# Expert weights stored in four 5 KB runs per partition, one store on another queue, two units loaded and squared earlier

## The chip, the cores and the metric

The kernel runs on one NeuronCore of a Trainium2 chip as one program. Its time is the device time in microseconds; of the kernel before there are three runs, median 822.89 us (820.84 to 823.64).
## The reference

Three stages follow each other. A gated linear recurrence over 4 x 8 heads of 768 steps gives 3072 rows of 320 numbers. Each row goes through one of eight experts (two products with a relu between them, 320 to 1024 to 320), the one with the largest logit, and is scaled by its gate. Then a dense layer follows (320 to 2048 to 320).

```python
for t in range(S):                      # recurrence, for every batch and head
    m_new = np.maximum(f_gate[:, :, t] + m, i_gate[:, :, t])
    f_stab = np.exp(f_gate[:, :, t] + m - m_new)
    i_stab = np.exp(i_gate[:, :, t] - m_new)
    C = f_stab * C + i_stab * outer(v_t, k_t);  n = f_stab * n + i_stab * k_t
    y[:, :, t] = sigmoid(o_gate_t) * (C @ q_t) / max(abs(n . q_t), 1)
# experts
expert_idx = np.argmax(x @ w_gate, axis=1); gate_w = softmax(x @ w_gate)[expert_idx]
for e in range(8):
    out[mask] = gate_w[mask, None] * (np.maximum(x[mask] @ w1[e], 0) @ w2[e])
# dense layer
h = x @ w_in; g = np.maximum(0.01 * h, h); return g @ w_out
```

## The kernel before

Everything is in single precision at the borders; weights and activations of the experts and of the dense layer are split in two halves of 16 bits each (a high and a low part), and each product is made of three 16-bit products.

**The weights.** There are ten weight units: 0 to 7 are the experts in the order in which they will be used, 8 and 9 the two halves of the dense layer. A unit goes through four steps, always in five parts (three of its first matrix, two of its second): it is *loaded* as f32 into one half of `stage` (even units into half 0, odd ones into half 1); ACT *squares* each part and keeps the row sums (`square`); TensorE adds the sums over partitions (`sums`), and DVE makes the unit's scale from them (`scale`); ACT writes the *high* parts and DVE the *low* parts into one of four 16-bit buffers `slot0` to `slot3`. Units 0 and 1 stay in slots 0 and 1. Units 2 to 7 are built in other slots and *stored* to `d_w` in DRAM, 20 KB in each of 128 partitions: unit 2 and 3 in two pieces of 10 KB (`store_A`, `store_B` on the sync queue, during the recurrence), 4 to 7 in one piece (`store_unit` on ACT's queue). The sync engine fetches them back into slots 0 and 1 in two pieces of 10 KB per partition when the expert two before them is done (the last loop of the sync block).

**The pairs.** The expert stage walks 31 pairs (tile of 128 rows, expert), in the order of the experts. In step p TensorE makes the first product of pair p (`h_product`, 64 matmuls), the second of pair p - 1 (`y_product`, 24 matmuls), and turns the rows of pair p + 2 (`x_turn`, 3 matmuls). Both products stand twice in the code, for slot 0 and slot 1, behind a branch on the parity of the expert. ACT copies out the high parts (`h_high`, `x_high`), scales the next rows (`x_cast`); DVE makes the low parts (`h_low`, `x_low`), the scale of the rows (`x_scale`) and adds the result (`y_add`). GpSimd gathers the rows of later pairs.

**What sets the order.** The steps of the weight units are spread over the pairs by tables at the end of the file. `PAIR_SQ` names the squares that ACT does in `jobs(p)`, `PAIR_HI` the high parts there, `PAIR_LO` the low parts that DVE does in its `jobs(p)`, `PAIR_SCALE` the pair before which TensorE adds the sums (and DVE makes the scale), `PAIR_STORE` and `PAIR_LOAD` the pairs at whose end ACT issues a store or a load (`keep(p)`). On ACT a step p is `h_high(p)`, `jobs(p)`, `x_cast(p + 3)`, `x_high(p + 2)`, `keep(p)`; on DVE `h_low(p)`, `x_scale(p + 3)`, `jobs(p)`, `y_gate` and `y_add` of p - 1, `x_low(p + 2)`. A load of unit x waits until the low parts of unit x - 2 are made, since they read the same half of `stage`. TensorE's pairs are loops of two pairs each, cut at the keys of `PAIR_SCALE` (3 to 9, 9 to 13, 13 to 23, 23 to 29). After the pairs comes the dense layer, six groups of four tiles, in which nothing of this is left but the two units in slots 2 and 3.

Of the kernel before, what the change touches and what calls it, by code (L numbers as in the profile page):

```python
# [24 lines left out]
F16 = mybir.dt.float16  # L25
# [8 lines left out]
P = 128  # L34
# [14 lines left out]
NF = FE // P  # L49
# [15 lines left out]
def build(nc, qkT, k_in, v_in, o_in, ig, fg, wg_in, wA, wB, out):  # L65
    ctx = ExitStack()
    with ctx:
# [3 lines left out]
        def dram(name, shape, dt):  # L71
            return nc.dram_tensor(name, shape, dt, kind="Internal").ap()
# [4 lines left out]

        d_parts = dram("d_parts", (6, BH, S), BF16)
        d_wl = dram("d_wl", (BH, NC), F32)
        d_w = dram("d_w", (NE, P, 5 * FE + NF * 2 * DM), F16)  # L80
        d_x = dram("d_x", (NTOK, DM), F32)

        slot = [sb(f"slot{i}", [P, 5 * FE + NF * 2 * DM], F16) for i in range(4)]
        slotA = [t[:, 0:5 * FE] for t in slot]
        slotB = [t[:, 5 * FE:] for t in slot]
# [100 lines left out]
        hi_done, lo_done = sem("hi_done"), sem("lo_done")  # L187
        stored = [sem(f"stored{k}") if k >= 2 else None for k in range(NE)]
# [9 lines left out]
        wA_landed = [sem(f"wA_landed{i}") for i in range(2)]  # L198
        wB_landed = [sem(f"wB_landed{i}") for i in range(2)]
# [120 lines left out]
        def _(sp):  # L320
# [13 lines left out]
            def load_B(x):  # L334

                h = x % 2
                r = row_of(sp, x)
                sp.dma_start(stB[h].rearrange("p (m e) -> p m e", m=NF // 2),
                             wB[ds(r, 1)].rearrange("a (m p r) d -> p (a m) (r d)", m=NF // 2, p=P)).then_inc(stgB_landed[h], 16)

            def store_A(x):

                sp.wait_ge(lo_done, lows_until(x, 3))
                sp.dma_start(d_w[x - 2, :, 0:5 * FE], slotA[SLOT[x]][:, :]).then_inc(stored[x], 16)

            def store_B(x):

                sp.wait_ge(lo_done, lows_until(x))
                sp.dma_start(d_w[x - 2, :, 5 * FE:], slotB[SLOT[x]][:, :]).then_inc(stored[x], 16)

            def load_k(c, b):
                i = buf(c, b)
# [37 lines left out]
            for g in range(NG):  # L390
                r = heads(g) * D
# [80 lines left out]
            sp.wait_ge(lo_done, lows_until(1))  # L472
            load_A(5)
            load_B(5)
            sp.wait_ge(rt_tab, 1)
            for e in range(2, NE):
                last = sp.value_load(tab_last[0:1, e - 2:e - 1], min_val=0, max_val=NPAIR)
                sp.wait_ge(stored[e], stores(e))
                sp.wait_ge(m_h, 2 * (last + 1))
                sp.dma_start(slotA[e % 2][:, :], d_w[e - 2, :, 0:5 * FE]).then_inc(wA_landed[e % 2], 16)  # L480
                sp.wait_ge(m_o, last + 1)
                sp.dma_start(slotB[e % 2][:, :], d_w[e - 2, :, 5 * FE:]).then_inc(wB_landed[e % 2], 16)

        @block.gpsimd
# [215 lines left out]
        def _(act):  # L701
# [188 lines left out]
            def store_unit(x):  # L890

                act.wait_ge(lo_done, lows_until(x))
                act.dma_start(d_w[x - 2], slot[SLOT[x]][:, :]).then_inc(stored[x], 16)

            def x_high(p, i):
                act.wait_ge(mtr, p + 1)
# [603 lines left out]
        def _(pe):  # L1500
# [373 lines left out]
SLOT = (0, 1, 0, 1, 2, 3, 2, 3, 2, 3)  # L1874
# [28 lines left out]
PAIR_LO = {0: ((4, 0), (4, 1)), 1: ((4, 2), (4, 3)), 2: ((4, 4), (5, 0)), 3: ((5, 1), (5, 2)), 4: ((5, 3), (5, 4)),  # L1903
# [90 lines left out]
```

## Time and profile before

| | |
|---|---|
| median of 3 runs | 822.89 us |
| the profiled execution | 821.72 us |
| its span | 820.0 us |
| TensorE busy | 748.0 us, 91% |
| VectorE (DVE) busy | 518.3 us, 63% |
| ScalarE (ACT) busy | 415.9 us, 51% |
| GpSimd (POOL) busy | 192.4 us, 23% |
| DMA | 95.77 MB in 35879 packets |

The profiled execution took 1.17 us less than the median. The recurrence lies at about 12 to 190 us of the span, the choice of experts at 190 to 217, the pairs at 217 to 465, and the dense layer from there to the end. In the page a group of rows names line, engine, operation, what is written and read, and how often; "issue" is time in which an engine waited for nothing that the profile shows; ACTq and SPq are the sequencers of ACT and SP, on which DMAs are issued.

### The profile page before, as it was taken

To read this page: it belongs to the slowest core of one execution; us is meant where nothing else is said; L and a number is where in the kernel's file an instruction comes from. 1 tells how busy PE (TensorE), PEld (TensorE's weight loads), DVE (VectorE), ACT (ScalarE), POOL (GpSimd) and SP (SyncE) were. 2 spreads that over 40 slices of the span, in tenths; PEclk is the share of its full clock that TensorE was granted. 3 is DMA by queue.
4 is the path that set the end of the run, shared out by engine and by line. 5 is a ranking of instruction groups with operands and counts; after the bars stand their busy time and mean duration, and the time that the engine had idled before them with its cause. 6 is when DMAs were issued, how large, how long until landed. Compare 5 with 4: busy or idle time off the path is not lost.

```text
span 820.0 us, 17971 instructions
## 1 busy us (share of the span) xinstructions
PE 748.0 (91%) x6435; PEld 554.9 (68%) x6436; DVE 518.3 (63%) x1346; ACT 415.9 (51%) x811; POOL 192.4 (23%) x286
## 2 busy tenths in 40 slices
PE   4899999993697989799999899999999999999994
PEld 3688889882486878687888756556565555565552
DVE  7868898997876545565567665555465455554441
ACT  4578777778652266554656223343443433434332
POOL 4468787782311001010100000020010100100101
PEclk9999999997798989999999999999999999999997
DMA  6889979732415974478330000000000000000000
GB/s 198 225 233 298 335 239 318 226 128 80 127 59 215 354 253 147 162 282 338 109 139 0 2 1 1 1 33 1 1 33 1 33 0 0 32 0 0 33 2 32
DMA packets 35879, 95.77 MB, mean 117 GB/s; under 512 B 7102, under 2 KB 19582, under 8 KB 33246
## 3 DMA queue, kind: packets, MB, share of 16 engines
q1 hardware_dynamic: 28434, 63.71, 24.6%
q10 hardware_dynamic: 4732, 22.10, 7.5%
q0 software_dynamic: 2640, 9.01, 3.3%
q8 instruction: 43, 0.70, 0.4%
q14 instruction: 30, 0.25, 0.1%
HBM read 70.92 MB, written 23.89 MB: 116 GB/s over the span
## 4 chain that ended last, share of the span: by engine, by line
PE 79%; DVE 5%; ACT 5%; DMA 4%; issue 4%; SPq 1%; POOL 1%; ACTq 0%; DVEq 0%; POOLq 0%
PE bank L1669 33%; PE bank L1806 19%; PE bank L1703 10%; PE bank L1532 4%; PE bank L1556 4%; DMA stage<-wA 2%; ACT xw L777 1%; PE bank L1578 1%; PE bank L1542 1%; PE bank L1548 1%; PE bank L1659 1%; DMA slot<-qkT 1%; DMA d_x<-og 1%; PE bank L1522 1%; PE bank L1524 1%
## 5 line engine op out<-in xcount | busy, mean ns | idle before, releaser
L1669 PE MATMUL bank<-stage,slot 128*128 128x512 f16 x768 | 181.1, 379 | 0.0
L1806 PE MATMUL bank<-slot,dec 128*128 128x320 f16 x768 | 159.1, 299 | 0.0
L1669 PE MATMUL bank<-qbd,slot 128*128 128x128 f16 x1984 | 122.5, 225 | 13.7 <-issue 9.3
L1669 PEld LDWEIGHTS bank<-qbd,slot 128*128 128x128 f16 x1984 | 118.4, 101 | 17.2 <-issue 16.8
L1669 PEld LDWEIGHTS bank<-stage,slot 128*128 128x128 f16 x768 | 75.1, 98 | 74.3 <-DVE stage L1464 0.3
L1468 DVE TENSOR_TENSOR qk<-stage,dec 128x512 f16<-128x512 f32 x96 | 66.4, 692 | 85.1 <-ACT dec L964 85.1
L1806 PE MATMUL bank<-slot,qk 128*128 128x320 f16 x384 | 114.8, 299 | 0.0
L964 ACT CAST dec<-stage 128x512 f16<-128x512 f32 x96 | 59.4, 619 | 101.1 <-PE bank L1806 74.5
L693 POOL DMA_INDIRECT out<-stage,tok_i x24 | 23.6, 983 | 369.5 <-ACT stage L975 365.6
L1464 DVE TENSOR_TENSOR stage<-bank,stage 128x512 f32<-128x512 f32 x96 | 66.2, 690 | 67.0 <-ACT stage L958 66.0
L958 ACT ACTIVATE stage<-bank 128x512 f32<-128x512 f32 x96 | 57.3, 597 | 97.2 <-PE bank L1669 96.2
L1703 PE MATMUL bank<-slot,emov 128*128 128x320 f16 x496 | 102.0, 299 | 4.3 <-DVE esta L1364 2.4
L1806 PEld LDWEIGHTS bank<-slot,dec 128*128 128x128 f16 x768 | 75.1, 98 | 44.3 <-DVE qk L1468 0.2
L905 ACT ACTIVATE emov<-bank 128x512 f16<-128x512 f32 x62 | 36.8, 597 | 92.0 <-PE bank L1669 88.5
L1703 PE MATMUL bank<-slot,esta 128*128 128x320 f16 x248 | 74.2, 299 | 0.0
L1364 DVE SCALAR_TENSOR_TENSOR esta<-bank,emov 128x512 f16<-128x512 f32 x62 | 42.1, 689 | 47.2 <-ACT emov L905 46.8
L1125 DVE SCALAR_TENSOR_TENSOR slot<-stage,wsc,slot 128x1024 f16<-128x1024 f32 (+2 forms) x50 | 71.0, 1430 | 0.4
L793 ACT ACTIVATE slot<-stage,wsc 128x1024 f16<-128x1024 f32 (+1 forms) x50 | 62.2, 1276 | 0.7 <-DVE winvp L1105 0.7
L1703 PEld LDWEIGHTS bank<-slot,emov 128*128 128x128 f16 x496 | 46.9, 98 | 22.1 <-issue 5.6
L1806 PEld LDWEIGHTS bank<-slot,qk 128*128 128x128 f16 x384 | 37.6, 98 | 14.6
L1132 DVE TENSOR_TENSOR dec<-bank,dec 128x384 f32<-128x384 f32 (+1 forms) x72 | 36.4, 506 | 14.4 <-ACT dec L835 13.5
L607 POOL TENSOR_TENSOR own<-state,bdm 120x123 f32<-120x123 f32 x60 | 41.6, 705 | 5.7 <-PE bank L1548 4.7
(268 smaller groups left out, 1187.6 us busy)
## 6 DMA issues: line engine op xcount, KB each, us to landing
slot<-d_w SPq DMA_DIRECT2D x12, 1280.0 KB, 6.5
d_w<-slot ACTq DMA_DIRECT2D x4, 2560.0 KB, 11.2
stage<-wB SPq DMA_DIRECT2D x6, 1280.0 KB, 9.0
stage<-wA SPq DMA_DIRECT2D x6, 1024.0 KB
d_w<-slot SPq DMA_DIRECT2D x4, 1280.0 KB, 8.3
stage<-wB ACTq DMA_DIRECT2D x4, 1280.0 KB, 13.2
qk<-qkT SPq DMA_DIRECT2D x12, 360.0 KB, 5.9
slot<-qkT SPq DMA_DIRECT2D x12, 360.0 KB, 7.8
```

The costliest lines, as they stand in the source:

```text
L607: nc.gpsimd.tensor_tensor(own[u % 3][0:GH * D, :], state[0:GH * D, b, g, :], bdm[0:GH * D, :], ALU.mult).then_inc(st_own, 1)
L793: a.activation(o_, t, ACT.Copy, scale=sc).then_inc(hi_done, 1)
L905: a.activation(hh[i][:, q * 512:(q + 1) * 512], bank[2 * i + q][:, :], ACT.Relu).then_inc(m_hh, 1)
L958: a.activation(ft[f % 2], bank[f % 2][:, :], ACT.Copy, scale=0.01).then_inc(f_t, 1)
L964: a.copy(fhi[f % 2], fgl[f % 2]).then_inc(f_hi, 1)
L1125: v.scalar_tensor_tensor(o_, x, sc, h_, ALU.mult, ALU.subtract).then_inc(lo_done, 1)
L1364: v.scalar_tensor_tensor(hl[i][:, q * 512:(q + 1) * 512], bank[2 * i + q][:, :], 0.0, hh[i][:, q * 512:(q + 1) * 512], ALU.max, ALU.subtra ...
L1464: v.tensor_tensor(fgl[f % 2], bank[f % 2][:, :], ft[f % 2], ALU.max).then_inc(f_g, 1)
L1468: v.tensor_tensor(flo[f % 2], fgl[f % 2], fhi[f % 2], ALU.subtract).then_inc(f_lo, 1)
L1669: ins = t_.matmul(pf, a[:, col:col + P], x(k), start=(q == 0), stop=(q == len(ops) - 1))
L1703: ins = t_.matmul(bank[4 + i][:, 0:DM], x[i][:, f * P:(f + 1) * P], slotB[s][:, c0:c0 + DM], start=(f == 0 and q == 0), stop=(f == NF - 1 ...
L1806: ins = t_.matmul(bank[4 + q][:, 0:DM], x[f % 2][:, q * P:(q + 1) * P], slotB[2 + f // NF][:, c0:c0 + DM], start=(f == 0 and z == 0), stop ...
```

## The change

Three things change. `d_w` is laid out as four runs of 2560 numbers (5 KB) per partition, all partitions of a run together, and each store and each fetch back moves rows of 5 KB (`WRUN`, `in_runs`, `kept`). The store of unit 4 goes from ACT's `keep(2)` to the sync engine, ahead of its fetches. The tables move the steps of units 4 to 8.

```diff
-        d_w = dram("d_w", (NE, P, 5 * FE + NF * 2 * DM), F16)
+        d_w = dram("d_w", (NE, 4, P, WRUN), F16)
...
+        def in_runs(t):
+            return t.rearrange("p (r w) -> p r w", w=WRUN)
+        def kept(e, lo, hi):
+            return d_w[e - 2, lo:hi].rearrange("r p w -> p r w")
...
                 sp.wait_ge(lo_done, lows_until(x, 3))
-                sp.dma_start(d_w[x - 2, :, 0:5 * FE], slotA[SLOT[x]][:, :]).then_inc(stored[x], 16)
+                sp.dma_start(kept(x, 0, 2), in_runs(slotA[SLOT[x]])).then_inc(stored[x], 16)
...
                 sp.wait_ge(lo_done, lows_until(x))
-                sp.dma_start(d_w[x - 2, :, 5 * FE:], slotB[SLOT[x]][:, :]).then_inc(stored[x], 16)
+                sp.dma_start(kept(x, 2, 4), in_runs(slotB[SLOT[x]])).then_inc(stored[x], 16)
...
             load_A(5)
             load_B(5)
+            sp.wait_ge(lo_done, lows_until(4))
+            sp.dma_start(kept(4, 0, 4), in_runs(slot[SLOT[4]])).then_inc(stored[4], 16)
             sp.wait_ge(rt_tab, 1)
             for e in range(2, NE):
                 last = sp.value_load(tab_last[0:1, e - 2:e - 1], min_val=0, max_val=NPAIR)
                 sp.wait_ge(stored[e], stores(e))
                 sp.wait_ge(m_h, 2 * (last + 1))
-                sp.dma_start(slotA[e % 2][:, :], d_w[e - 2, :, 0:5 * FE]).then_inc(wA_landed[e % 2], 16)
+                sp.dma_start(in_runs(slotA[e % 2]), kept(e, 0, 2)).then_inc(wA_landed[e % 2], 16)
                 sp.wait_ge(m_o, last + 1)
-                sp.dma_start(slotB[e % 2][:, :], d_w[e - 2, :, 5 * FE:]).then_inc(wB_landed[e % 2], 16)
+                sp.dma_start(in_runs(slotB[e % 2]), kept(e, 2, 4)).then_inc(wB_landed[e % 2], 16)
...
             def store_unit(x):
                 act.wait_ge(lo_done, lows_until(x))
-                act.dma_start(d_w[x - 2], slot[SLOT[x]][:, :]).then_inc(stored[x], 16)
+                act.dma_start(kept(x, 0, 4), in_runs(slot[SLOT[x]])).then_inc(stored[x], 16)
...
-PAIR_SCALE = {9: 6, 13: 7, 23: 8}
+PAIR_SCALE = {9: 6, 15: 7, 23: 8}
...
-PAIR_STORE = {2: 4, 4: 5, 13: 6, 17: 7}
-PAIR_LOAD = {5: 6, 8: 7, 14: 8, 18: 9}
+PAIR_STORE = {4: 5, 13: 6, 18: 7}
+PAIR_LOAD = {3: 6, 6: 7, 14: 8, 18: 9}
```

`PAIR_SQ`, `PAIR_HI` and `PAIR_LO` change with them. The squares of unit 6 go from pairs 7 (three) and 8 (two) to pairs 5, 6 (two each) and 7 (one); those of unit 7 from pairs 11 (two) and 12 (three) to one in each of the pairs 9 to 13; those of unit 8 from pairs 16 and 17 to 17, 18 and 19. The high parts of unit 7 go from pairs 13 to 15 to 15 to 17, its low parts from 14 to 17 to 15 to 18. Of unit 4's low parts four now lie in pair 0 (before: two) and the fifth in pair 1 (before: pair 2).

What stands on ACT before, from the load of unit 6 at the end of pair 5 (rows `DMA stage<-wA`) to the squares of that unit (`xw,sq<-stage`) in pairs 7 and 8. Each pair begins with `emov<-bank 128x512` (`h_high`) and has `qk<-` (`x_cast`) and `qbd<-bank` (`x_high`).

```order
L883 DMA stage<-wA 128x2x1024
L886 ISA
L886 DMA stage<-wA 64x1024 x2
L887 DMA stage<-wB 128x4x640
L905 ACTIVATE emov<-bank 128x512 [waits m_h] x2
L920 ACTIVATE qk<-num,sxs 128x320 [waits mtr,xs_scale]
L921 ACTIVATE qk<-num,sxs 128x64
L899 CAST qbd<-bank 128x384 [waits m_h,mtr]
L905 ACTIVATE emov<-bank 128x512 [waits m_h] x2
L777 ACTIVATE xw,sq<-stage 128x1024 [waits sq_done,stgA_landed0]
L777 ACTIVATE xw,sq<-stage 128x1024 [waits sq_done] x2
```

The same stretch of ACT in the changed kernel: the load of unit 6 at the end of pair 3, the store of unit 5 at the end of pair 4, and the first squares in pair 5.

```order
L893 DMA stage<-wA 128x2x1024
L896 ISA
L896 DMA stage<-wA 64x1024 x2
L897 DMA stage<-wB 128x4x640
L915 ACTIVATE emov<-bank 128x512 [waits m_h] x2
L930 ACTIVATE qk<-og,sxs 128x320 [waits mtr,xs_scale]
L931 ACTIVATE qk<-og,sxs 128x64
L909 CAST qbd<-bank 128x384 [waits m_h,mtr]
L903 DMA d_w<-slot 128x4x2560 [waits lo_done]
L915 ACTIVATE emov<-bank 128x512 [waits m_h] x2
L787 ACTIVATE xw,sq<-stage 128x1024 [waits sq_done,stgA_landed0]
L787 ACTIVATE xw,sq<-stage 128x1024 [waits sq_done]
```

One whole pair lies between the load and the first square in both; the store of unit 5, which stood before the load, now stands behind it in ACT's queue.

On ACT before pair 13, before: the squares of unit 7 in pairs 11 and 12, ahead of the high parts of the same unit (`slot<-stage`, waiting for its scale, `sc_chain`) in pair 13.

```order
L777 ACTIVATE xw,sq<-stage 128x1024 [waits sq_done,stgA_landed1]
L777 ACTIVATE xw,sq<-stage 128x1024 [waits sq_done]
L920 ACTIVATE qk<-og,sxs 128x320 [waits mtr,xs_scale]
L921 ACTIVATE qk<-og,sxs 128x64
L899 CAST qbd<-bank 128x384 [waits m_h,mtr]
L905 ACTIVATE emov<-bank 128x512 [waits m_h] x2
L777 ACTIVATE xw,sq<-stage 128x1024 [waits sq_done]
L777 ACTIVATE xw,sq<-stage 128x1280 [waits sq_done,stgB_landed1]
L777 ACTIVATE xw,sq<-stage 128x1280 [waits sq_done]
```

In the changed kernel, from the last square of unit 7 in pair 13 to its first high part in pair 15:

```order
L787 ACTIVATE xw,sq<-stage 128x1280 [waits sq_done]
L930 ACTIVATE qk<-num,sxs 128x320 [waits mtr,xs_scale]
L931 ACTIVATE qk<-num,sxs 128x64
L909 CAST qbd<-bank 128x384 [waits m_h,mtr]
L903 DMA d_w<-slot 128x4x2560 [waits lo_done]
L915 ACTIVATE emov<-bank 128x512 [waits m_h] x2
L930 ACTIVATE qk<-num,sxs 128x320 [waits mtr,xs_scale]
L931 ACTIVATE qk<-num,sxs 128x64
L909 CAST qbd<-bank 128x384 [waits m_h,mtr]
```

A pair now lies between the last square and the sum that TensorE makes of them, where before the sum stood right behind it.

On DVE in pairs 0 and 1, before: the low parts of units 4 and 5 (`slot<-stage,wsc,slot`), the gates of the pairs (`gmt<-bank`), and `x_low` of pair 2 (`qbd<-bank,qbd`), for which TensorE's pair 2 waits.

```order
L1354 RECIPROCAL sxs<-sxi 128x1 [waits xs_chain]
L1125 SCALAR_TENSOR_TENSOR slot<-stage,wsc,slot 128x1024 [waits hi_done] x2
L1320 TENSOR_REDUCE gmt<-bank 128x31 [waits rt_gate]
L1359 TENSOR_TENSOR qbd<-bank,qbd 128x384 [waits m_xh,rt]
L1364 SCALAR_TENSOR_TENSOR esta<-bank,emov 128x512 [waits m_hh] x2
```

And in the changed kernel:

```order
L1135 SCALAR_TENSOR_TENSOR slot<-stage,wsc,slot 128x1024 [waits hi_done] x2
L1135 SCALAR_TENSOR_TENSOR slot<-stage,wsc,slot 64x1024 [waits hi_done]
L1135 SCALAR_TENSOR_TENSOR slot<-stage,wsc,slot 128x4x320 [waits hi_done]
L1330 TENSOR_REDUCE gmt<-bank 128x31 [waits rt_gate]
L1369 TENSOR_TENSOR qbd<-bank,qbd 128x384 [waits m_xh,rt]
L1374 SCALAR_TENSOR_TENSOR esta<-bank,emov 128x512 [waits m_hh] x2
```

Two more low parts stand ahead of the gates and of `x_low`.

## Rows read from the trace of the kernel before

**Rows 1.** The page: busy times and the granted clock in 40 slices.
```profile
PE 748.0 (91%) x6435; PEld 554.9 (68%) x6436; DVE 518.3 (63%) x1346; ACT 415.9 (51%) x811; POOL 192.4 (23%) x286
PEclk9999999997798989999999999999999999999997
```
**Rows 2.** Timeline of PE, clean pairs: start, duration, operation, count, idle before.
```profile
352.08 3.74 PE L1669 MATMUL bank<-qbd,slot 128*128 128x128 f16 x64 [0.21 <-issue]
...
373.72 3.74 PE L1669 MATMUL bank<-qbd,slot 128*128 128x128 f16 x64
```
**Rows 3.** Timeline of PE, pairs 2 to 6 and 8 to 9.
```profile
234.72 0.49 PE L1659 MATMUL bank<-ident,qk 128*128 128x128 f32 x3
...
242.20 3.74 PE L1669 MATMUL bank<-qbd,slot 128*128 128x128 f16 x64
...
253.73 6.07 PE L1669 MATMUL bank<-qbd,slot 128*128 128x128 f16 x64 [4.20 <-issue]
...
271.78 3.75 PE L1669 MATMUL bank<-qbd,slot 128*128 128x128 f16 x64 [0.88 <-issue]
...
286.16 3.74 PE L1669 MATMUL bank<-qbd,slot 128*128 128x128 f16 x64
...
295.04 0.36 PE L1591 MATMUL bank<-sq,onesf 128*128 128x5 f32 x2 [1.55 <-ACT xw L777]
297.23 6.49 PE L1669 MATMUL bank<-qbd,slot 128*128 128x128 f16 x64 [1.83 <-DVE qbd L1359]
```
**Rows 4.** Timeline of PE, pairs 12 to 14 and 19.
```profile
323.21 3.74 PE L1669 MATMUL bank<-qbd,slot 128*128 128x128 f16 x64
...
334.06 5.20 PE L1669 MATMUL bank<-qbd,slot 128*128 128x128 f16 x64 [2.09 <-DVE qbd L1359]
...
348.11 0.44 PE L1703 MATMUL bank<-slot,emov 128*128 128x320 f16 x2 [1.69 <-DVE esta L1364]
...
382.74 3.75 PE L1669 MATMUL bank<-qbd,slot 128*128 128x128 f16 x64 [1.70 <-issue]
```
**Rows 5.** Timeline of ACT: first and last of four stores, load and square of unit 6.
```profile
243.57 0.36 ACTq L893 DMA_DIRECT2D d_w<-slot  x1
...
250.47 0.46 ACT L899 CAST qbd<-bank 128x384 f16<-128x384 f32 x1
...
272.47 0.45 ACTq L883 DMA_DIRECT2D stage<-wA  x1
...
286.71 1.06 ACT L777 ACTIVATE xw<-stage 128x1024 bf16<-128x1024 f32 x1 [3.33 <-DMA stage<-wA]
...
374.29 0.34 ACTq L893 DMA_DIRECT2D d_w<-slot  x1
```
**Rows 6.** DMA view: packets, and issues with sizes and time to landing.
```profile
DMA packets 35879, 95.77 MB, mean 117 GB/s; under 512 B 7102, under 2 KB 19582, under 8 KB 33246
...
q8 instruction: 43, 0.70, 0.4%
q14 instruction: 30, 0.25, 0.1%
...
slot<-d_w SPq DMA_DIRECT2D x12, 1280.0 KB, 6.5
d_w<-slot ACTq DMA_DIRECT2D x4, 2560.0 KB, 11.2
```
**Rows 7.** Windows: busy times, granted clock, DMA share, GB/s.
```profile
250.00:260.00 10.00, 6.27 (x67) 6.20 (x68) 4.13 (x6) 1.69 (x5) 0.94 (x1) 0.66 0.51 197
280.00:290.00 10.00, 10.00 (x143) 9.05 (x140) 3.90 (x11) 4.42 (x7) 0.10 (x1) 1.00 1.01 358
```
**Rows 8.** Timeline of DVE, pairs 0 and 1: low parts, `x_low` of pair 2.
```profile
227.39 2.46 DVE L1125 SCALAR_TENSOR_TENSOR slot<-stage,wsc,slot 128x1024 f16<-128x1024 f32 x2
...
231.91 0.56 DVE L1359 TENSOR_TENSOR qbd<-bank,qbd 128x384 f16<-128x384 f32 x1 [0.70 <-ACT qbd L899]
...
234.84 2.87 DVE L1125 SCALAR_TENSOR_TENSOR slot<-stage,wsc,slot 64x1024 f16<-64x1024 f32 x2
```

More of the change, by code:

```diff
@@ L1857 @@
 NBUF = 4
+WRUN = 2560
 EARLY = 4
@@ L1894 @@
 STABLE = {(1, 0): (1, 2), (1, 1): (2, 3), (1, 2): (3, 4), (2, 0): (4, 5), (2, 1): (5, NC)}
-PAIR_SQ = {7: ((6, 0), (6, 1), (6, 2)), 8: ((6, 3), (6, 4)),
-           11: ((7, 0), (7, 1)), 12: ((7, 2), (7, 3), (7, 4)), 16: ((8, 0), (8, 1)), 17: ((8, 2), (8, 3), (8, 4)),
-           20: ((9, 0), (9, 1), (9, 2)), 21: ((9, 3), (9, 4))}
-PAIR_SCALE = {9: 6, 13: 7, 23: 8}
+PAIR_SQ = {5: ((6, 0), (6, 1)), 6: ((6, 2), (6, 3)), 7: ((6, 4),),
+           9: ((7, 0),), 10: ((7, 1),), 11: ((7, 2),), 12: ((7, 3),), 13: ((7, 4),), 17: ((8, 0),), 18: ((8, 1), (8, 2)),
+           19: ((8, 3), (8, 4)), 20: ((9, 0), (9, 1), (9, 2)), 21: ((9, 3), (9, 4))}
+PAIR_SCALE = {9: 6, 15: 7, 23: 8}
 PAIR_HI = {0: ((5, 0), (5, 1)), 1: ((5, 2), (5, 3)), 2: ((5, 4),),
[2 rows of a table removed]
[2 rows of a table added]
            23: ((8, 0), (8, 1)), 24: ((8, 2), (8, 3)), 25: ((8, 4), (9, 0)), 26: ((9, 1), (9, 2)), 27: ((9, 3), (9, 4))}
-PAIR_LO = {0: ((4, 0), (4, 1)), 1: ((4, 2), (4, 3)), 2: ((4, 4), (5, 0)), 3: ((5, 1), (5, 2)), 4: ((5, 3), (5, 4)),
+PAIR_LO = {0: ((4, 0), (4, 1), (4, 2), (4, 3)), 1: ((4, 4), (5, 0)), 2: ((5, 1), (5, 2)), 3: ((5, 3),), 4: ((5, 4),),
            9: ((6, 0),), 10: ((6, 1),), 11: ((6, 2),), 12: ((6, 3),), 13: ((6, 4),),
[1 row of a table removed]
[1 row of a table added]
            23: ((8, 0),), 24: ((8, 1), (8, 2)), 25: ((8, 3),), 26: ((8, 4), (9, 0)), 27: ((9, 1), (9, 2)),
            28: ((9, 3), (9, 4))}
-PAIR_STORE = {2: 4, 4: 5, 13: 6, 17: 7}
-PAIR_LOAD = {5: 6, 8: 7, 14: 8, 18: 9}
+PAIR_STORE = {4: 5, 13: 6, 18: 7}
+PAIR_LOAD = {3: 6, 6: 7, 14: 8, 18: 9}
 TOK_AT = 21
```

6 rows, old and new, of tables (PAIR_HI, PAIR_LO) are left out of this document.

## The prediction

> **What bounds the kernel now.** I read the page first, then the timeline of TensorE (PE) pair by pair, then the timelines of ACT and DVE where PE is late, and last the DMA view. PE is busy 91% of the span, and the row of granted clocks is full but for a dent between 180 and 330 us [rows 1]: what is lost lies in the expert stage, not in the dense layer. A clean pair, from the first product of pair 15 (352.08) to that of pair 18 (373.72), takes 21.64 / 3 = 7.21 us, in which the 64 matmuls of a first product take 3.74 [rows 2]. From pair 3 (242.20) to pair 18 there are 15 pairs; 131.52 - 15 x 7.21 = 23.4 us too many, and pair 19 waits 1.70 more: 25 us lost [rows 2 to 4]. They have two kinds of cause.
>
> **Two sums that wait for ACT.** Before pair 9 PE adds the squares of unit 6, and waits 1.55 us for them; the first product then starts another 1.83 us late, since PE came to its register work only behind that wait [rows 3]. Of ACT one sees why: the first square of unit 6 waited 3.33 us for a load that was issued at 272.47 and landed at 286.7, 14.2 us later [rows 5], with the DMA engines 101% busy from 280 to 290 [rows 7]. Pair 8 to 9 takes 297.23 - 286.16 = 11.07, 3.86 too many, and the product of pair 9 runs at the lower clock in part, 6.49 against 3.74, 2.75 more [rows 3]: 6.6 us. Before pair 13 the same with unit 7, whose squares stand in pair 12 itself: 334.06 - 323.21 = 10.85, 3.64 too many, and 5.20 against 3.74, 1.46 more [rows 4]: 5.1 us.
>
> **Four waits that no engine explains.** Pair 4 waits 4.20 us [rows 3], pair 6 0.88 [rows 3], the second product behind pair 14's first 1.69 and pair 19 1.70 [rows 4]; the releaser given for the third, a low part of pair 14, is none that `y_product(13)` waits for. Each begins 3 to 7 us after ACT issued one of its four stores (the first at 243.57, the last at 374.29 [rows 5], the others at 265.3 and 343.3): at 249.5, 270.9, 346.4 and 381.0. A store takes 11.2 us to land [rows 6], so all four lie inside one. Beside other traffic that keeps the DMA engines as busy, 280 to 290 at 1.01, PE is busy 10.00 of 10.00 [rows 7]. What the stores have that the rest lacks is rows of 20 KB: 35879 - 33246 = 2633 packets are of 8 KB or more, and 12 fetches, 4 stores of unit halves and 4 whole stores at 128 each make 2560 of them, the 43 + 30 instruction fetches the other 73 [rows 6]. An instruction fetch is 0.70 MB / 43 = 16 KB in one packet [rows 6]; both products stand behind a branch, so PE needs such fetches in every pair. I read the four waits as fetches, or register loads, held up behind 20 KB packets: 4.20 + 0.88 + 1.69 + 1.70 = 8.47 us. The longest cost the clock too: 0.66 of it granted from 250 to 260 [rows 7], partly at 1.2 GHz, and 64 matmuls in 6.07 instead of 3.74 [rows 3], 2.33 more. Together 10.8 us.
>
> On this the Trainium skill agrees in kind: "Runtime: NRT & Kernel Launch" (Instruction fetch mechanics) says that a taken branch out of the window stops the engine for a DMA fetch, and "DMA: Bandwidth & Descriptors" (Queues, rings and completion order) that a DMA engine changes queues only at packet boundaries. The second page's section "Issuing engines are not separate DMA queues" speaks against a part of this change: a store moved to another issuer runs on the same 16 engines and saves only issue time; by it the fifth unit's store on the sync queue is worth nothing for itself, and what it may bring is its earlier start. The sum below gives it nothing.
>
> **The change part by part.**
>
> *Squares of unit 6 two pairs sooner.* The load goes out at the end of pair 3, when `x_high(5)` is done, at 250.9 [rows 5]; its first square stands in pair 5. If pair 4 no longer waits (249.5), pair 5 starts at about 256.7, and ACT comes to the square behind its copy of the product, some 4.2 us later, at 260.9: 10 us after the issue. The load took 14.2 us where store 5's tail and two fetches ran beside it; now the fetch of unit 2 (issued about 246, 6.5 us to land) runs beside its start, and the store of unit 5, about 258, stands behind it in ACT's queue. I expect 9 to 12 us. ACT may wait 5 us more there without delaying PE: `x_high(7)` would be ready at about T5 + 8.1 and is needed at T5 + 14.3. So the point of no cost is a landing of 15 us. Sum 6 then needs nothing that isn't done 8 us earlier, and PE passes it as it passes other waits. Gain 6.6; from below, if the sum still waits, 0.
>
> *Squares of unit 7 spread over pairs 9 to 13, sum at pair 15.* The last lies one pair ahead of the sum. Each pair gets one square beside at most two high parts, on an ACT with room: what stood in a pair before (three squares) was more. Gain 5.1; nothing else in the pair is late behind it. The low parts end in pair 18 instead of 17, and store 7 and load 9 are issued one behind the other; unit 7 is fetched 5 pairs later and unit 9 squared 2 pairs later, so both have over 14 us.
>
> *Runs of 5 KB.* The number of bytes stays; 3584 packets are added (1536 for four whole stores, 512 for the halves, 1536 for the fetches). What a store of 5 KB rows costs PE is not in the trace. From above: the four waits stay, 0. From below: they go, with the clock, 10.8. The nearest row is the busy window with 10 KB rows and no wait [rows 7], nearer to the gain. I take a quarter of the waits as left, as the packet is a quarter as long: 3/4 x 8.47 + 2.33 = 8.7. A cost of more, smaller packets I put at 0: over half the packets are already under 2 KB [rows 6].
>
> *Unit 4's low parts and its store.* DVE makes four in pair 0, not two: one over 64 partitions and one of 1280 columns more, 2.87 us for the like pair [rows 8]. They end at 229.85 + 2.87 = 232.7; with the short sum of the gates behind them, `x_low(2)` starts at about 233.0 instead of 231.91 and ends at 233.6 [rows 8]. PE turns the next rows at 234.72 [rows 3]; 1.1 us are left. In pairs 1 and 2 DVE is as much behind and has as much left. Cost 0; without that cover 1 us a pair. The store starts at about 237.6 instead of 243.57 and has landed at 249 when pair 4 begins. The sync engine waits there for low parts; behind it stands only the fetch of unit 2, which must wait for pair 3 anyway (246).
>
> *What it adds.* Between 250 and 272 the load of unit 6, the store of unit 5 and the second fetch of unit 2 lie closer than before, with pairs 4 to 7 beside them. The 0.88 us of pair 6 is the nearest row for such a crowd [rows 3]; I add 1.0 us.
>
> **The sum**, from the profiled execution: 821.72 - 6.6 - 5.1 - 8.7 + 1.0 = 802.3 us. That execution lay 1.17 below the median of 822.89; against the median I predict 803.5 us.
>
> **Rivals.**
>
> 1. *The four waits stay.* They come from reading SBUF or from the branch, not from long rows. For it: pair 4 is the first that takes the other branch. Against it: pairs 11 and 18 switch too and don't wait. Only 6.6 + 5.1 go: 821.72 - 11.7 + 1.0 = 811.0, against the median 812.2.
> 2. *The load of unit 6 is late again, two pairs sooner.* The 3.33 us of ACT come back in pair 5 or 6, now beyond its 5 us of room, and a pair starts late with a slow product: 2 to 4 us and 2.8 us for the clock. 803.5 + 5 to 7 = 809 to 810.
> 3. *It gets slower.* One mechanism: rows of 5 KB slow load, store and fetch in the crowd of 250 to 272 so far that ACT stands in pair 5 at the first square. It costs nothing up to 15 us of landing and then its full excess, plus 2.8 us for the clock; it eats the 19.4 us of gain only from 15 + 16.6 = 32 us, over twice the 14.2 that the most crowded load took [rows 5]. Then 823 to 828.
> 4. *All four waits and the added crowd come to nothing:* 821.72 - 6.6 - 5.1 - 10.8 = 799.2, against the median 800.4.
>
> **How the numbers follow.** Forecast 0.58 (own range 800 to 807), rival 1 0.15, rival 2 0.12, rival 4 0.08, rival 3 0.04, and 0.03 that gains and new waits cancel to within 0.3% (2.5 us, about what a measurement of this kernel can tell). The range takes in rivals 1, 2 and 4: 798 to 813. Faster 0.93, same 0.03, slower 0.04.
>
> **What would show it.** Right: pair 9 and pair 15 (first product) start within 7.5 us of the one before, and no product of 64 matmuls from pair 4 to 18 takes over 4 us; the windows from 250 to 340 have a granted clock of 1.00; the four stores have no wait of PE over 1 us inside them; about 39460 packets, of which 73 of 8 KB or more. Wrong: a wait "issue" of several us near pair 4 with a store of 5 KB rows in flight (rival 1); an ACT square of unit 6 waiting for `stage<-wA` in pair 5 and a late pair 7 (rival 2); a load that needs over 20 us (rival 3). The recurrence and the dense layer should take as long as before; a gain there would be none of mine.

## The result: 0.7% faster, some 28% of the gain forecast

The changed kernel takes 818.18 us in the median of 9 runs (813.51 to 819.57), beside 823.64 for the kernel before on the same chip (820.84 to 827.13): a ratio of 0.9927, 95% interval 0.9906 to 0.9948. The forecast was 803.5 us, with a range of 798 to 813. Faster is right; it was to bring 19.4 us, and 5.5 came (823.64 less 818.18). The profiled execution has a span of 817.7 us. Lines of the changed kernel that stand behind the diff are 10 higher (`h_product` is L1679, `y_product` L1713).

From the page of the changed kernel, the rows that answer to [rows 1, 6]:

```profile
PE 747.7 (91%) x6435; PEld 552.2 (68%) x6436; DVE 518.1 (63%) x1346; ACT 415.4 (51%) x811; POOL 193.2 (24%) x286
...
PEclk9999999997799999989999999999999999999997
...
DMA packets 39463, 95.77 MB, mean 117 GB/s; under 512 B 7102, under 2 KB 19582, under 8 KB 39390
...
q8 instruction: 43, 0.70, 0.4%
q14 instruction: 30, 0.25, 0.1%
```

The packets are as forecast (39463, of them 73 of 8 KB or more). The dents of the clock in slices 13 and 15 (246 to 266 and 287 to 308 us) are gone, and a new one stands in slice 18, at 350 us. Where the time went is told best by the starts of the first products of the pairs, taken from the timeline of TensorE (PE), whose rows for the new trouble are these (start, duration, idle time before and its releaser):

```profile
246.73 3.75 PE L1679 MATMUL bank<-qbd,slot 128*128 128x128 f16 x64 [1.90 <-issue]
...
291.33 0.28 PE L1601 MATMUL bank<-sq,onesf 128*128 128x5 f32 x2
291.53 0.67 PE L1679 MATMUL bank<-qbd,slot 128*128 128x128 f16 x9
...
335.50 0.28 PE L1601 MATMUL bank<-sq,onesf 128*128 128x5 f32 x2
336.96 3.75 PE L1679 MATMUL bank<-qbd,slot 128*128 128x128 f16 x64 [1.18 <-issue]
...
345.80 3.75 PE L1679 MATMUL bank<-qbd,slot 128*128 128x128 f16 x64 [1.51 <-issue]
353.30 0.71 PE L1713 MATMUL bank<-slot,emov 128*128 128x320 f16 x2 [3.76 <-issue]
...
359.55 3.74 PE L1679 MATMUL bank<-qbd,slot 128*128 128x128 f16 x64
...
400.26 5.09 PE L1679 MATMUL bank<-qbd,slot 128*128 128x128 f16 x64 [1.40 <-DVE esta L1374]
```

Both sums are passed without a wait: unit 6 at 291.33 (1.55 and 1.83 us lost there before [rows 3]) and unit 7 at 335.50. But pairs 15 and 16 now wait three times, 1.18 + 1.51 + 3.76 = 6.45 us, and the longest wait costs the clock as well. Pair 3 waits 1.90 us where it waited for nothing before; this lies inside the 46.86 us of pairs 2 to 8 below. The windows of the changed kernel (busy times, granted clock, DMA share, GB/s):

```profile
345.00:350.00 5.00, 3.75 (x64) 3.58 (x64) 1.71 (x3) 1.02 (x2) 0.46 (x1) 1.00 0.99 307
350.00:355.00 5.00, 1.70 (x7) 1.02 (x8) 4.39 (x9) 3.21 (x5) 1.52 (x1) 0.69 0.07 21
355.00:360.00 5.00, 5.00 (x31) 3.25 (x29) 0.47 (x1) 0.25 (x1) 0.37 (x1) 0.62 0.11 33
```

PE was idle from 349.5 to 353.3 and then ran its second product with a granted clock of 0.62, 0.71 us for two matmuls where 0.43 is usual. The DMA engines were full until 350 (load of unit 8, issued 335.70) and all but empty after it.

A table from the starts of first products, in us; a clean pair is 7.21:

| from the start of pair to pair | before | after | forecast of the difference | difference |
|---|---|---|---|---|
| 2 to 8 | 51.12 | 46.86 | -5.1 (waits of pairs 4 and 6, clock, +1.0) | -4.26 |
| 8 to 11 | 29.88 | 22.45 | -6.6 (sum of unit 6) | -7.43 |
| 11 to 12 | 7.17 | 7.17 | 0 | 0 |
| 12 to 15 | 28.87 | 23.17 | -6.4 (sum of unit 7, wait in pair 14) | -5.70 |
| 15 to 18 | 21.64 | 29.75 | 0 | +8.11 |
| 18 to 23 | 38.06 | 42.23 | -1.3 (wait of pair 19) | +4.17 |
| 2 to 23 | 176.74 | 171.63 | -19.4 | -5.11 |

Up to pair 15 the change brought 17.4 us of 18.1. The miss lies behind it. (Pair 2 starts at 237.31, before at 235.04; over the traces of this study it lies between 235.0 and 239.6, and most of that arises ahead of the pairs, where traces of kernels with the same code differ by up to 4 us, so the rest of this text compares pairs 2 to 23, and medians. One part of it is the change's own: from the first product of pair 0 to that of pair 2 it is 14.47 us, before 14.03.)

### The profile page after: what moved, and what is told of

It reads as the page before. It is cut to its first block, busy times and chain, and to the rows that moved or that the text cites. A ratio compares the mean times of both kernels' runs of the same rounds, so it can differ in the third digit from the quotient of the medians.

```text
span 817.7 us, 17971 instructions
## 1 busy us (share of the span) xinstructions
PE 747.7 (91%) x6435; PEld 552.2 (68%) x6436; DVE 518.1 (63%) x1346; ACT 415.4 (51%) x811; POOL 193.2 (24%) x286
## 2 busy tenths in 40 slices
DMA packets 39463, 95.77 MB, mean 117 GB/s; under 512 B 7102, under 2 KB 19582, under 8 KB 39390
## 4 chain that ended last, share of the span: by engine, by line
PE 80%; DVE 7%; DMA 5%; issue 4%; ACT 2%; SPq 1%; POOL 1%; ACTq 0%; DVEq 0%; POOLq 0%
PE bank L1679 33%; PE bank L1816 19%; PE bank L1713 11%; PE bank L1542 4%; PE bank L1566 4%; DMA stage<-wA 2%; PE bank L1588 1%; PE bank L1552 1%; PE bank L1558 1%; PE bank L1669 1%; DMA slot<-qkT 1%; DMA d_x<-og 1%; PE bank L1532 1%; PE bank L1534 1%; PE bank L1793 1%
## 5 line engine op out<-in xcount | busy, mean ns | idle before, releaser
L1679 PE MATMUL bank<-stage,slot 128*128 128x512 f16 x768 | 181.1, 379 | 0.0
L1679 PE MATMUL bank<-qbd,slot 128*128 128x128 f16 x1984 | 117.5, 220 | 10.0 <-issue 8.3
L1679 PEld LDWEIGHTS bank<-stage,slot 128*128 128x128 f16 x768 | 75.1, 98 | 74.3 <-DVE stage L1474 0.2
L1679 PEld LDWEIGHTS bank<-qbd,slot 128*128 128x128 f16 x1984 | 113.2, 98 | 13.9 <-issue 13.5
L1713 PE MATMUL bank<-slot,emov 128*128 128x320 f16 x496 | 104.3, 304 | 7.0 <-issue 6.3
L1713 PE MATMUL bank<-slot,esta 128*128 128x320 f16 x248 | 75.3, 304 | 0.0
L1713 PEld LDWEIGHTS bank<-slot,emov 128*128 128x128 f16 x496 | 47.6, 99 | 26.2 <-issue 8.7
```

Source lines behind the costliest of these rows:

```text
L1679: ins = t_.matmul(pf, a[:, col:col + P], x(k), start=(q == 0), stop=(q == len(ops) - 1))
L1713: ins = t_.matmul(bank[4 + i][:, 0:DM], x[i][:, f * P:(f + 1) * P], slotB[s][:, c0:c0 + DM], start=(f == 0 and q == 0), stop=(f == NF - 1 ...
```

## The theory: new code under full DMA engines

PE's program holds four copies of the pair loop, since each sum of squares ends one loop and starts the next: pairs 3 to 8, 9 up to the sum of unit 7, on to 22, and 23 on. Theory N: PE fetches its code only where it has not run yet, so in the first pass (two pairs) of each copy; if the DMA engines are full then, that fetch is late, whatever the row length. Moving the sum of unit 7 from pair 13 to 15 moved the start of the third copy onto the load of unit 8, issued at 335.70. The DMA view, cut to windows, shows the code packets of PE's queue (q8). From 332 to 356 us of the changed kernel:

```profile
q8 instruction: 3, 0.05, 0.9%
```

and none from 356 to 400, while the five pairs 17 to 21 run, in which only the second instruction queue, q14 [rows 6], has a packet:

```profile
q14 instruction: 1, 0.01, 0.0%
```

The view puts a packet where it starts. In narrow windows the three start at 342.3, 350.2 and 353.4. The first two belong to waits of PE, the one that ends at 345.80 and the one that ends at 353.30; the third starts when PE is already running again. Each wait goes on for some 2 us behind its packet (of about 1 us), the longest with the DMA engines all but empty (share 0.07 from 350): the full engines can have made that packet late, but not the time behind it.

The rivals were the prediction's term C (the rows decide), and R: a full DMA system stops PE in any pass. No packet of q8 lies near the first wait (1.18 us, ahead of pair 15; none from 304.5 to 342): theory N doesn't explain it, and it comes back below.

## Experiments

Ratios are to the kernel before on the same chip, with 95% intervals. "Time 2 to 23" is from the first product of pair 2 to that of pair 23, in the profiled execution.

**1. The rows alone** (e1_runs_alone), on the kernel before: `d_w` in runs of 5 KB, with `kept` and `in_runs` for stores and fetches.

> The kernel before with the 5 KB rows and nothing else. Theory N (the waits are fetches of TensorE's own code, which happen only in the first two pairs of each of the four copies of the pair loop, and last long when the DMA engines are full, whatever the rows): the waits before h_product of pairs 4, 10, 13/14 stay in sum within 3 us of the 8.5 us of before, and the time is 0.998 to 1.004 of before. The prediction's term C (row length sets the waits): at least three of the four waits fall under 1 us, and the time is 0.987 to 0.993 of before.

Measured: 821.68 us, 0.9974 (0.9953 to 0.9996). Ahead of pair 4, timeline of PE:

```profile
255.45 5.37 PE L1677 MATMUL bank<-qbd,slot 128*128 128x128 f16 x64 [3.87 <-issue]
```

3.87 us where it was 4.20 [rows 3]; pair 14 waits 1.09 (1.69 [rows 4]) and pair 19 1.69 (1.70). Pairs 2 to 8 take 50.18 us (51.12), all other stretches the same within 0.06. Rows of 5 KB are worth about 1 us in the trace and, by the interval of the ratio, 0.3 to 3.9 us in the time, not 8.7. The ratio lies between the two forecasts, 0.0006 outside theory N's and further from term C's; only one wait of four is under 1 us (pair 6, 0.58, before 0.88), where term C wanted three.

**2. The changed kernel with the old rows** (e2_long_rows):

```diff
-        d_w = dram("d_w", (NE, 4, P, WRUN), F16)
+        d_w = dram("d_w", (NE, P, 5 * FE + NF * 2 * DM), F16)
```

(and the stores and fetches without `kept` and `in_runs`)

> The changed kernel with its rows put back to the old length (20 KB stores, 10 KB fetches), all else as changed. Theory N: the same time as the changed kernel within 0.3% (816 to 821 us), waits at pairs 15 to 17 of 5 to 8 us as there. Term C: 6 to 10 us slower than the changed kernel (824 to 828 us), with waits of 2 us and more that the changed kernel does not have.

Measured: 819.44 us, 0.994 (0.9916 to 0.9964), beside 0.9927: no difference to be told. Waits in pairs 15 and 16 of 1.25 + 1.78 + 3.56 us, as with 5 KB rows. Term C has fallen from both sides.

**3. The sum of unit 7 back at pair 13** (e3_sum7_at_13), the load of unit 8 left where it is:

```diff
-PAIR_SCALE = {9: 6, 15: 7, 23: 8}
+PAIR_SCALE = {9: 6, 13: 7, 23: 8}
...
-PAIR_STORE = {4: 5, 13: 6, 18: 7}
+PAIR_STORE = {4: 5, 13: 6, 17: 7}
```

(squares of unit 7 done by pair 12, high parts from 13, low parts from 14)

> The changed kernel with the sum of unit 7 put back ahead of pair 13, with its high and low parts and its store (keep(17)) where they were before; load of 8 still in keep(14). So the third copy of the loop is entered at pair 13, two pairs ahead of the load of unit 8. Theory N: the 6.5 us of waits and about 2.8 us of low clock in pairs 15 to 17 go, 1 to 4 us come at pairs 13 and 14 (store of unit 6 and a fetch are in flight there): 4 to 8 us faster than the changed kernel (810 to 814 us). Rival (the waits follow the load and store, wherever the loop's copy begins): pairs 15 to 17 lose the same 6 us, the time is that of the changed kernel.

Measured: 810.59 us, 0.9848 (0.9821 to 0.9876). Pairs 15 to 18 take 21.64 us, to the hundredth as before the change, with the same load in flight: it does not stop PE in a second pass. Pairs 13 to 15 wait 2.02 + 1.00 + 0.61 us now (12 to 15 takes 25.74, not 23.17). Pairs 18 to 23 take 37.66 us, not 42.23: the store of unit 7, a pair earlier here, no longer stands directly ahead of the load of unit 9, which lands in 13.8 us (issued 367.52) where it took 18.3. Against the changed kernel the two ratios are 6.5 us apart; the profiled run, 807.4, is the second fastest of seven.

**4. The load of unit 8 two pairs later** (e4_load8_later), the sum left at pair 15:

```diff
-PAIR_LOAD = {3: 6, 6: 7, 14: 8, 18: 9}
+PAIR_LOAD = {3: 6, 6: 7, 16: 8, 18: 9}
```

(squares of unit 8 in pairs 18 to 20, of unit 9 in 21 and 22)

> The changed kernel with the load of unit 8 two pairs later (keep(16), squares in pairs 18 to 20) and the squares of unit 9 one pair later (21, 22). The third copy of the loop is then entered at pair 15 with only the store of unit 6 just ended. Theory N: pairs 15 to 17 lose at most 2 us (of 6.5 us and 2.8 us of clock), and the wait for the landing of unit 9 in pair 21 shrinks by about 5 us: 6 to 11 us faster than the changed kernel (807 to 812 us). Rival (the waits follow the load wherever it goes): waits of about 6 us now at pairs 17 to 19, the time falls by at most 4 us, from unit 9 alone.

Measured: 809.41 us, 0.9823 (0.9792 to 0.9854). Timeline of PE, first products of pairs 15 to 18:

```profile
336.24 3.75 PE L1679 MATMUL bank<-qbd,slot 128*128 128x128 f16 x64 [1.17 <-issue]
343.44 3.75 PE L1679 MATMUL bank<-qbd,slot 128*128 128x128 f16 x64
...
351.50 3.75 PE L1679 MATMUL bank<-qbd,slot 128*128 128x128 f16 x64
358.67 3.74 PE L1679 MATMUL bank<-qbd,slot 128*128 128x128 f16 x64
```

22.43 us from pair 15 to 18, not 29.75. The load runs in pairs 17 and 18 (DMA share 1.03 from 355 to 365, PE busy 5.00 of 5.00 in both windows): the waits did not follow it. What stays is the first one: 1.17 us ahead of pair 15, as in the changed kernel, with no packet of q8 from 304 to 340. So 1.51 + 3.76 us and the lower clock belong to the load of unit 8, and the 1.18 us do not. Against the changed kernel the two ratios are 8.6 us apart.

**5 to 7. New code and a crowd, each alone and together**, on the kernel of experiment 4. The crowd:

```diff
+                if p == 10:
+                    act.wait_ge(stored[2], stores(2))
+                    for n in range(2):
+                        act.dma_start(d_junk[n].rearrange("r p w -> p r w"), kept(2, 0, 4)).then_inc(junk, 16)
+                if p == 13:
+                    act.wait_ge(junk, 32)
```

The new code:

```diff
+                if p == 15:
+                    pairs(at, 11)
+                    at = 11
```

Both (s1_copy_and_crowd):

> On e4_load8_later. Added: the loop of pairs 9 to 14 is written as two loops (9 and 10, 11 to 14), so that pairs 11 and 12 run through a copy of the code not run before; and at the end of ScalarE's work of pair 10 two copies of 2.6 MB each from DRAM to DRAM in 5 KB rows that nobody reads, so that the DMA engines are full through pairs 11 to 13. Theory N (TensorE waits for its own code where it is new and the DMA engines are full): 3 to 8 us of waits without a releasing engine at pairs 11 and 12. Rival R (the crowd itself stalls register loads or instructions in any iteration): the same waits as in s2_crowd_alone.

The crowd alone (s2_crowd_alone):

> e4_load8_later with the two copies of 2.6 MB in pairs 11 to 13 alone; the pairs 11 and 12 are the second pass through the loop entered at pair 9. Theory N: under 1 us of waits in pairs 11 to 13 and the time of e4_load8_later within 0.3%. Rival R: as many microseconds of waits as in s1_copy_and_crowd (3 to 8), and the time by these longer.

The new code alone (s3_copy_alone):

> e4_load8_later with the loop split at pair 11 alone. Theory N: the new copy is fetched while the DMA engines are nearly idle, with waits of 0 to 1 us at pairs 11 and 12 (as 0.2 us at pair 23), time as e4_load8_later within 0.3%. A second rival (a new copy costs its waits however idle the DMA engines are): 3 us and more.

| | no crowd | crowd |
|---|---|---|
| pairs 11, 12 in their second pass | 30.33 us | 30.28 us |
| pairs 11, 12 in new code | 30.96 us | 35.56 us |

(start of pair 11 to start of pair 15.) Each alone costs nothing or 0.6 us, both together 5.2. Timeline of PE with both:

```profile
305.83 3.75 PE L1687 MATMUL bank<-qbd,slot 128*128 128x128 f16 x64 [0.31 <-issue]
...
313.00 3.62 PE L1687 MATMUL bank<-qbd,slot 128*128 128x128 f16 x62
319.75 0.37 PE L1687 MATMUL bank<-qbd,slot 128*128 128x128 f16 x2 [3.13 <-issue]
320.55 0.71 PE L1721 MATMUL bank<-slot,emov 128*128 128x320 f16 x2 [0.43 <-issue]
```

PE stops in the middle of a product, after 62 of 64 matmuls, where no semaphore is waited for; the windows beside it, with both:

```profile
312.00:316.00 4.00, 4.00 (x64) 3.84 (x62) 2.99 (x6) 2.27 (x6) 0.95 (x1) 1.00 1.05 315
316.00:320.00 4.00, 0.87 (x14) 0.57 (x11) 0.32 (x1) 0.00 (x0) 0.00 (x0) 0.98 0.93 288
320.00:324.00 4.00, 3.57 (x18) 2.12 (x17) 3.07 (x7) 3.79 (x6) 0.00 (x0) 0.60 1.00 398
```

and with the crowd alone:

```profile
312.00:316.00 4.00, 4.00 (x40) 3.19 (x38) 3.21 (x8) 3.97 (x7) 0.24 (x1) 1.00 1.02 369
316.00:320.00 4.00, 4.00 (x64) 3.70 (x62) 2.00 (x4) 1.52 (x3) 0.71 (x1) 1.00 1.02 330
```

With both, a packet of q8 starts in the 1 us from 317 and PE goes on at 319.75; with the crowd alone q8 has no packet between 305 and 336. And the page with the new code alone:

```profile
q8 instruction: 46, 0.75, 0.4%
```

Three packets more than 43, about the length of one copy of a two-pair loop. The pairs that run are the same, so if each pass fetched its code, nothing would have been added. Medians: both 812.97 us, 0.9897 (0.9869 to 0.9926); crowd 810.69, 0.9865 (0.9839 to 0.9891); new code 811.36, 0.9859 (0.9836 to 0.9882); beside 0.9823 (0.9792 to 0.9854) for neither. That the crowd and the new code alone would be within 0.3% of that is a slight miss (0.4% by the middle values, intervals overlap); the crowd pushed the store of unit 6 further into pairs 15 and 16, which took 1.1 us more to pair 18.

**8. Both, with rows of 20 KB in the crowd** (s4_long_crowd):

```diff
-        d_junk = dram("d_junk", (2, 4, P, WRUN), F16)
+        d_junk = dram("d_junk", (2, P, 4 * WRUN + 32), F16)
```

> s1_copy_and_crowd with the two copies of 2.6 MB laid out in 128 rows of 20 KB each, not 512 of 5 KB: the row length alone, in front of a first pass through new code. Term C of the prediction (code fetches queue behind rows, so the wait grows with the row): pairs 11 and 12 lose two to four times what s1_copy_and_crowd lost there (5.1 us against s2_crowd_alone), 10 us and more, and the time is 5 us or more longer. Theory N as sharpened by the first results (full engines and new code decide, the row length hardly): the same loss within 2 us, the time of s1_copy_and_crowd within 0.3%.

Measured: 814.43 us, 0.9896 (0.9855 to 0.9936), and 36.01 us from pair 11 to 15. The wait stands behind the same 62 matmuls:

```profile
321.16 0.40 PE L1688 MATMUL bank<-qbd,slot 128*128 128x128 f16 x2 [3.64 <-issue]
```

3.64 us where rows of 5 KB gave 3.13, one trace each. Even these 0.5 us may be no effect of the row: the wait behind the first product of pair 16 reads 3.76, 3.68 and 4.10 us in three kernels with 5 KB rows (the changed one, experiments 9 and 10) and 3.56 with the long ones (experiment 2). The two medians are the same (0.9896 and 0.9897). Term C is worth at most that.

**9. The store of unit 4 back on ScalarE's queue** (u1_store4_by_act) (`PAIR_STORE = {2: 4, 4: 5, 13: 6, 18: 7}`, the sync queue's two lines gone), on the changed kernel.

> The changed kernel with the store of unit 4 back on ScalarE's queue after pair 2. The prediction put this part at 0: the time of the changed kernel within 0.3% (816 to 821 us). Rival: the store starts some 4 us later and lies in pairs 3 and 4, the first pass through the first copy of the loop, where the fetch of the third expert is in flight too: 1 to 3 us slower, with more waits there.

Measured: 822.07 us, 0.9989 (0.9971 to 1.0008), so it is slower than the changed kernel by more than the rival's 1 to 3 us, 3.9 by the medians. Pairs 2 to 8 take 51.40 us, not 46.86. Timeline of PE at pair 4:

```profile
254.63 0.56 PE L1677 MATMUL bank<-qbd,slot 128*128 128x128 f16 x7 [3.78 <-DVE qbd L1367]
```

The `x_low` named as releaser is that of pair 5; the one that pair 4 needs ended at 248.6, and the code packet of q8 starts in the 1 us from 251 (in the kernel before, in the 1 us from 250). The 4.20 us of before are back, with rows of 5 KB and full DMA engines (share 1.02 from 248 to 252). What removed them was that the store starts at 239.16 and not at 243.7, and leaves the engines before pair 4 is reached (DMA share 1.01 from 242 to 246, 0.34 from 248 to 250 in the changed kernel). It is no pure gain: the 1.90 us ahead of pair 3 are its price. The prediction costed this part at nothing.

**10. Loads and squares of units 6 and 7 as before** (u2_loads_as_before) (`PAIR_LOAD = {5: 6, 8: 7, 14: 8, 18: 9}`), sum of unit 7 left at pair 15.

> The changed kernel with the loads of units 6 and 7 after pairs 5 and 8 again (squares of 6 in pairs 7 and 8, of 7 in 11 to 13), the sum of 7 still ahead of pair 15. The prediction's term A: the sum of unit 6 waits for the squares again, 6 to 7 us slower than the changed kernel (824 to 826 us). Rival A2: part of the 8.3 us that the two instructions at this sum waited before was TensorE's own first pass through the copy of pair 9, and the load of 6 leaving pairs 3 and 4 gives some back: 3 to 5 us slower.

Measured: 825.64 us, 1.0036 (1.0017 to 1.0054), slower than before the change. Time 2 to 23 is 178.30 us against 171.63: 6.7 more. Of these 4.8 lie in pairs 8 to 11, 1.1 in pairs 2 to 8 and 0.6 in pairs 15 to 18. Timeline of PE, first products of pairs 9 and 10:

```profile
296.96 3.75 PE L1679 MATMUL bank<-qbd,slot 128*128 128x128 f16 x64 [1.84 <-DVE qbd L1369]
306.87 3.75 PE L1679 MATMUL bank<-qbd,slot 128*128 128x128 f16 x64 [2.58 <-DVE qbd L1369]
```

The total hits the 6.6 of the prediction, but the parts are others: no product here runs at the lower clock (2.75 us of the 6.6), and a packet of q8 starts in the 2 us from 303, just before the wait of pair 10, so the rival A2 has a share in it. The time (825.64) is inside the forecast, 7.5 us above the changed kernel.

**11. Experiment 4 with the store of unit 7 after pair 20** (e5_both) and the squares of units 8 and 9 in 18 to 21:

```diff
-PAIR_STORE = {4: 5, 13: 6, 18: 7}
+PAIR_STORE = {4: 5, 13: 6, 20: 7}
```

> e4_load8_later with the store of unit 7 after pair 20 and no longer just ahead of the load of unit 9, and the squares of units 8 and 9 done by pair 21. The load of unit 9 then lands in 8 to 10 us, not 18, the sum of units 8 and 9 is ready in pair 22, and pair 23 starts without its 1.81 us wait and its 1.6 us of low clock: 2 to 4 us faster than e4_load8_later, 805.5 to 808 us. Rival (the wait at pair 23 is this loop's own first pass): the same time as e4_load8_later.

Measured: 807.7 us (805.48 to 808.2), 0.9817 (0.9796 to 0.9838), the fastest of the study. Time 2 to 23 is 159.68 us, 1.7 less than experiment 4 (161.40). Pair 23 counts too, since it lost its wait and its slow product (1.81 us and 5.37 for 3.74 before): from pair 18 to pair 31 it takes 90.61 us against 94.08, 3.5 us less and inside the 2 to 4 foreseen. The medians don't show it (ratios 0.9817 and 0.9823, with intervals of 0.002 to 0.003 to each side). In the changed kernel the load of unit 9 goes out right behind the store of unit 7. Its timeline of ACT:

```profile
374.44 0.37 ACTq L903 DMA_DIRECT2D d_w<-slot  x1
374.85 0.52 ACTq L893 DMA_DIRECT2D stage<-wA  x1
...
393.11 1.06 ACT L787 ACTIVATE xw<-stage 128x1024 bf16<-128x1024 f32 x1 [6.40 <-DMA stage<-wA]
```

18.3 us to land; ACT waits 6.40, `x_high` is late and PE with it, at 398.31 and 400.26. Without the store ahead of it, no square waits.

**12. Experiment 11 with the store of unit 4 behind the fetch** (f1_store4_after_fetch) at 262 us.

> e5_both with the store of unit 4 issued by the sync queue behind the fetch of the third expert's second half (some 262 us) and no longer at 239 us, so that pairs 2 and 3 run without it. Theory N: the 1.76 us wait ahead of pair 3 shrinks to under 0.5 us; 1 to 2 us faster than e5_both (805.5 to 807 us), unless the crowd after 262 us delays the load of unit 7, which the squares of pair 9 would show. Rival (that wait is no fetch of code: it stays with the store elsewhere): the same wait, the same time as e5_both.

Measured: 808.78 us, 0.9827 (0.9803 to 0.9852), no gain. Timeline of PE:

```profile
247.24 3.74 PE L1680 MATMUL bank<-qbd,slot 128*128 128x128 f16 x64
...
300.90 3.75 PE L1680 MATMUL bank<-qbd,slot 128*128 128x128 f16 x64 [1.23 <-issue]
```

The wait ahead of pair 3 is gone, as forecast (1.76 in experiment 11), and 1.23 us stand at pair 10, in the first pass of the second copy, with a packet of q8 that starts in the 1 us from 298: the transfers that were put off fill the engines there (DMA share 0.76 from 295 to 300, 0.06 in experiment 11). Time 2 to 23 is 160.08 us.

## Why the prediction was wrong, step by step

- **The two sums.** Right: both are passed without a wait, and pairs 8 to 11 took 7.43 us less (forecast 6.6). That experiment 10 gives 6.7 us back is partly luck, as its parts are others. The gain of the sum of unit 7 (5.70 in pairs 12 to 15) was real and was lost again in pairs 15 to 18.
- **"I read the four waits as fetches, or register loads, held up behind 20 KB packets."** This step failed, and it is worth 8.7 us of the sum. Two of them are fetches as far as packets show (4.20 and 1.69; q8 packets start in the 1 us from 250 and in the 1 us from 345), the other two (0.88 and 1.70) have no packet near. And the row length is worth at most 0.5 us in 3 (experiment 8) and about 1 us in all (experiment 1). The step before it failed already: "both products stand behind a branch, so PE needs such fetches in every pair". It needs them in two pairs per copy. The Trainium skill ("Runtime: NRT & Kernel Launch", Instruction fetch mechanics) says that a taken branch out of the current two-page window stops the engine for a DMA fetch; these loops don't bear it out: each pass ends in a branch back over the whole body, five pairs ran from 356 to 400 us without one code packet, and a new copy of the loop added three packets with the same pairs run (experiment 7).
- **Unit 7, "nothing else in the pair is late behind it".** This was the dearest step. True for ACT and DVE; but with the sum the program text moved. The third copy of the loop now begins at pair 15 and meets the load of unit 8, kept at pair 14: +8.1 us in pairs 15 to 18. Experiments 3 and 4, which part the two in opposite ways, give 8.1 and 7.3 us of it back there (21.64 and 22.43 against 29.75). Each also changes the order around unit 9, so the 10.2 us of time 2 to 23 that either gives are not all of this cause.
- **Unit 9, "both have over 14 us".** It needed 18.3, since the store of unit 7 stands directly ahead of its load: most of the +4.2 us in pairs 18 to 23. With the store one pair earlier (experiment 3) these pairs take 37.66 us, with it two pairs later (experiment 11) 37.61, against 42.23.
- **The store on the sync queue, 0.** It is worth 4.0 us of time 2 to 23 (experiment 9: 175.62 against 171.63) and it, not the rows, took pair 4's wait away. The prediction had the store landed "when pair 4 begins" and priced that at nothing. That a move to another issuer saves only issue time (the Trainium skill, "DMA: Bandwidth & Descriptors", Issuing engines are not separate DMA queues) may still be so: what counted was a start 4.5 us earlier.
- **Unit 4's low parts, cost 0.** They cost 0.4 us ahead of pair 2 (14.47 us from the first product of pair 0 to that of pair 2, before 14.03), and in the traces of experiments 4 and 6, which take 15.37, PE waits 1.31 us there with DVE as the releaser: the 1.1 us of room was not always enough.
- **The added crowd, +1.0.** Pair 6 lost nothing. Pairs 2 to 8 as a whole came within 0.9 us of the forecast, by luck: the gain was the store's and not the rows', and the loss was at pair 3 and not at pair 6.
- **Rival 1** (the waits stay) was right that the long rows don't make them, and wrong that they stay: pair 4's went with the earlier store. Its time (812.2) missed too, since the prediction had no price for pairs 15 to 23. None of the rivals named a wait that would be new.

**What stays open.** Why a wait goes on for 1 to 2 us behind its code packet, with full engines or empty ones, was not tried. The wait of 1.18 us ahead of pair 15 (1.17 in experiment 4, 1.25 in experiment 11) is in a first pass but has no packet near. And some waits of 0.5 to 1.7 us stand outside first passes (pair 6 and pair 19 before [rows 3, 4], pair 19 in experiment 1, pair 22 in experiment 11), while transfers of 2.6 MB are under way. In the 1.70 us of pair 19 DVE waits as well, with nothing named as releaser; its timeline in the kernel before:

```profile
381.38 0.22 DVE L1370 SCALAR_TENSOR_TENSOR gmt<-gmt,sxi,winvp 128x1 f32<-128x1 f32 x1 [1.42 <-issue]
```

Both engines load registers from tables there. Ahead of pair 15 of the changed kernel DVE waits too (1.22 us, at 335.80). Whether these loads are slow was not tried; the crowd of experiment 6 did not show such a wait in pairs 11 to 14.

## What to carry to other kernels

Where a program has several copies of a loop, mark the first pass of each: there the engine fetches code, and large loads and stores in flight held it up for 3 to 5 us here (4.20 before, 1.51 + 3.76 in the changed kernel, 3.13 + 0.43 in experiment 5), and the clock with it. An event that splits a loop takes such a fetch along when it is moved, so check what transfers it lands on. And price a wait by when its transfer runs before pricing it by the shape of the transfer.

## What the runs showed of the hardware

- PE's code comes in packets of 16 KB (43 for 0.70 MB), and a copy of the loop brings its three once; a loop of some three packets stays and is run again without a fetch. The first pass of a new copy cost 0.6 us without the crowd (experiment 7) and 5.2 us with it (experiment 5): 3.13 + 0.43 of waits, the rest the lower clock.
- The granted clock fell to 0.60 of full speed in the 4 us behind an idle time of 3.1 us (experiment 5), to 0.62 behind one of 3.76 us, so mostly to 1.2 GHz of 2.4, and stayed at 1.00 in the windows around waits of 2.02 and 1.00 us in experiment 3.
- Five-KB rows and 20-KB rows moved 2.6 MB units with no difference in the kernel's time that experiments 2 and 8 can tell; experiment 1 has 0.3% for the short ones, with an interval that starts at 0.04%.
